# One pair of heads on GpSimd, and one probability unit, arranged anew in a fused attention and mixer kernel

## What is computed

```python
q_rot, k_rot = rotate(q), rotate(k)        # x1*cos - x2*sin, x1*sin + x2*cos
scores = scale * q_rot @ k_rot.T
attn = exp(scores - max(scores)); attn = attn / (sum(attn) + 1e-9)
x = attn @ v                               # all heads side by side: [4, 576, 512]
x = gated mixer(x; w_k, w_v, w_r)
x = token mixer and channel mixer(x; w_tok1, w_tok2, w_ch1, w_ch2)
```

## Time and profile before

| | us |
|---|---|
| median of 3 runs | 1166.11 (1163.17 to 1166.35) |
| the profiled execution | 1165.27 |
| its span in the profile | 1163.1 |
| first P0 that waits, head 2, to P0 of head 31: 29 slots | 28.42 to 476.35 |
| one slot, the mean | 15.45 |

### The profile page before, as it was taken

How to read it: one execution, slowest core, us unless ns; L and a number is a source line. 1 busy time by engine, 2 the same in 40 slices (tenths; PEclk the granted TensorE clock), 3 DMA queues, 4 the chain that set the end, 5 groups by cost and what they waited for, 6 DMA issues and landing times.

```text
span 1163.1 us, 21141 instructions
## 1 busy us (share of the span) xinstructions
PE 1016.8 (87%) x6976; PEld 961.7 (83%) x6976; DVE 636.4 (55%) x1232; ACT 537.0 (46%) x1280; POOL 298.0 (26%) x291
## 2 busy tenths in 40 slices
PE   4877777777777777879999999999999999999998
PEld 3766666666776666779999999988899999999997
DVE  5666666667666666779777777744522122212211
ACT  3666666666666666764444434435312112211210
POOL 4454555554544455442000000024200000000000
PEclk9888888998888888889999999999999999999999
DMA  3122222222222121111000000003000000000000
GB/s 81 38 60 58 60 57 52 53 60 60 60 42 42 40 39 31 22 47 62 1 0 0 0 0 0 0 28 108 28 1 21 21 1 20 20 20 0 20 20 20
DMA packets 93629, 37.70 MB, mean 32 GB/s; under 512 B 84000, under 2 KB 84896, under 8 KB 93600
## 3 DMA queue, kind: packets, MB, share of 16 engines
q1 hardware_dynamic: 93312, 37.00, 12.9%
q10 hardware_dynamic: 288, 0.33, 0.1%
HBM read 32.51 MB, written 4.80 MB: 32 GB/s over the span
## 4 chain that ended last, share of the span: by engine, by line
PE 66%; issue 14%; POOL 11%; ACT 5%; DVE 3%; POOLq 0%; DMA 0%; ACTq 0%; SPq 0%; DVEq 0%
PE psum L635 17%; PE psum L637 17%; PE psum L636 17%; PE psum L588 4%; POOL times_cos L481 3%; POOL times_sin L482 3%; PE psum L620 3%; PE psum L606 3%; POOL w_lo L501 2%; PE psum L572 2%; PE psum L626 2%; ACT probs L837 1%; ACT pT_hi L850 1%; POOL rot_q L486 1%; PE psum L723 1%
## 5 line engine op out<-in xcount | busy, mean ns | idle before, releaser
L1054 DVE TENSOR_REDUCE neg_max<-psum 128x1 f32<-128x576 f32 (+1 forms) x160 | 120.5, 753 | 120.8 <-PE psum L588 112.0
L1003 ACT ACTIVATE h_hi<-psum 128x288 fp32r<-128x288 f32 x96 | 39.5, 411 | 245.8 <-PE psum L637 245.8
L606 PE MATMUL psum<-ident,probs 128*128 128x128 f32 x800 | 137.9, 295 | 2.4 <-issue 2.3
L572 PE MATMUL psum<-ident,rot_q 128*128 128x128 f32 x96 | 24.7, 387 | 117.6 <-issue 109.1
L850 ACT ACTIVATE pT_hi<-psum 128x320 fp32r<-128x320 f32 (+3 forms) x224 | 100.7, 450 | 42.7 <-PE psum L606 38.9
L837 ACT ACTIVATE probs<-psum,neg_max 128x576 f32<-128x576 f32 (+1 forms) x160 | 118.0, 737 | 3.6 <-DVE neg_max L1054 2.0
L606 PEld LDWEIGHTS psum<-ident,probs 128*128 128x128 f32 x800 | 103.3, 151 | 17.9 <-issue 8.6
L588 PE MATMUL psum<-kT_hi,qT 128*128 128x288 f32 x320 | 111.3, 360 | 7.4 <-DVE kT_lo L1038 5.6
L572 PEld LDWEIGHTS psum<-ident,rot_q 128*128 128x128 f32 x96 | 14.4, 192 | 123.7 <-issue 123.7
L635 PE MATMUL psum<-u_hi,wc_hi 128*128 128x288 f32 x384 | 114.3, 298 | 0.2 <-DVEq L1239 0.2
L635 PE MATMUL psum<-h_hi,wc_hi 128*128 128x288 f32 x384 | 113.7, 296 | 0.0
(11 more groups left out here) (127 smaller groups left out, 2943.0 us busy)
## 6 DMA issues: line engine op xcount, KB each, us to landing
stage_w<-in_moe_w_ch_dram SPq DMA_DIRECT2D x8, 768.0 KB, 4.2
rb<-sum_rows SPq DMA_DIRECT2D x32, 144.0 KB, 3.6
out_dram<-stage_out SPq DMA_DIRECT2D x8, 576.0 KB, 3.7
raw_qk<-in_q_dram SPq DMA_DIRECT2D x32, 128.0 KB, 2.5
raw_qk<-in_k_dram SPq DMA_DIRECT2D x32, 128.0 KB, 2.3
raw_v<-in_v_dram SPq DMA_DIRECT2D x32, 128.0 KB
w_raw<-in_moe_w_k_dram SPq DMA_DIRECT2D x4, 512.0 KB, 5.0
w_raw<-in_moe_w_v_dram SPq DMA_DIRECT2D x4, 512.0 KB, 4.9
```

The lines of the kernel that those rows point to most:

```text
L572: t.transpose(prep_bank[:, p * P:(p + 1) * P], rot_q[i][:, 2 * p:2 * p + 2, :].rearrange("p a d -> p (a d)"), ident[:, :])
L606: ins = t.transpose(bank[:, at:at + P], probs[i][:, tile, at_key:at_key + P], ident[:, :])
L1054: d_.tensor_reduce(neg_max[0:m, at:at + 1], score_banks[at][0:m, :, 0:HALF], AX.XY, ALU.max, negate=True).then_inc(maxed, 1)
```

## The change

GpSimd's order in a pair becomes: rotation of head 2 it + 2, weights hi, split of the values of head 2 it, rotation of head 2 it + 3, weights lo, scaling of the pair before, split of the values of head 2 it + 1. `split_w1_hi` asks for `it` weight loads and no longer for `it + 1` (a piece is half a load). `WHOLE` is empty: unit 0 is split as the other seven are, so that each slot has an L0 (VectorE) and V0 is four FP32R matmuls. The three orders of a slot are written anew.

```diff
-    WHOLE = (0,)
+    WHOLE = ()
...
-    ORDER = steps("T0 T1 S0 P0 S1 T2 V0 T3 V1 S2 T4 V2 T5 S3 P1 T6 V3 T7 S4 V5 V4 V6 V7")
+    ORDER = steps("S0 T0 T1 S1 P0 T2 T3 V0 S2 T4 V1 T5 V2 S3 P1 T6 T7 V3 S4 V4 V6 V5 V7")
...
-    DVE_ORDER = steps("I0 M0 L0 L1 M1 P0 L2 P1 L3 M2 P2 L4 O0 L5 M3 L6 L7 M4 P3 O1")
+    DVE_ORDER = steps("M0 I0 L0 L1 M1 L2 P0 L3 M2 P1 P2 L4 L5 O0 M3 L6 L7 P3 M4 O1")
...
             def slots(it, n, scaling):
-                split_v(it, 0, 0)
                 rotate(it, 0, 2, False)
                 split_w1_hi(it, n)
+                split_v(it, 0, 0)
                 pool.wait_ge(w_hi, it + 1)
-                split_v(it, 1, 1)
+                rotate(it, 1, 3, False)
                 split_w1_lo(it)
-                rotate(it, 1, 3, False)
                 if scaling:
                     scale_x(it - 1)
+                split_v(it, 1, 1)
...
-                slots(it, it + 1, True)
+                slots(it, it, True)
...
-                if n == WHOLE[-1]:
+                if n == 0:
```

More of the change, by code:

```diff
@@ L60, in steps @@
         return [(x[0], int(x[1])) for x in text.split()]
-    ORDER = steps("T0 T1 S0 P0 S1 T2 V0 T3 V1 S2 T4 V2 T5 S3 P1 T6 V3 T7 S4 V5 V4 V6 V7")
-    ACT_ORDER = steps("H0 H1 P0 P1 P2 H2 E0 H3 E1 H4 O0 H5 E2 v0 H6 H7 P3 E3 O1 E4")
-    DVE_ORDER = steps("I0 M0 L0 L1 M1 P0 L2 P1 L3 M2 P2 L4 O0 L5 M3 L6 L7 M4 P3 O1")
+    ORDER = steps("S0 T0 T1 S1 P0 T2 T3 V0 S2 T4 V1 T5 V2 S3 P1 T6 T7 V3 S4 V4 V6 V5 V7")
+    ACT_ORDER = steps("H0 H1 E0 H2 P0 P1 H3 P2 E1 H4 v0 H5 O0 E2 H6 H7 P3 E3 O1 E4")
+    DVE_ORDER = steps("M0 I0 L0 L1 M1 L2 P0 L3 M2 P1 P2 L4 L5 O0 M3 L6 L7 P3 M4 O1")
     LAST_ORDER = steps("T0 T1 V0 V1 T2 T3 V2 T4 V3 K0 T5 V4 K1 T6 V5 K2 T7 V6 K3 V7")
```

## The result

| | us | ratio to the kernel before |
|---|---|---|
| before, median of 4 runs | 1166.23 | |
| changed, median of 4 runs | 1100.29 (1098.07 to 1101.30) | 0.9432 (0.9404 to 0.9461) |
| predicted | 1054 (1038 to 1086) | |

The direction was right and the size was not: 66 us gained where 112 were forecast, and the time lies above the forecast range. The profiled execution of the changed kernel took 1101.3 us, its span is 1099.3.

A forecast was written before the change was run, and what follows sets the result against it. GpSimd and the attention slot waited for each other, 15.45 us a slot; then VectorE would bind at 11.7. 29 x (15.45 - 11.7) = 108.8, plus 3.4, less 0.7, is 111.5 us saved: 1054, range 1038 to 1086.

The forecast's parts named there:

- a ring of waits: Attention slot: P0, v0, split of the values, rotation, next P0; 15.45 us a slot, whole wait at P0 claimed gone.
- the turn that you forecast: Attention slot without the wait at P0, as long as VectorE needs: floor 11.08 plus 0.6 idle, 11.7 us (11.1 to 12.3).

## What to carry to other kernels

When a ring of waits is cut, the next one is the longest of all the rings, those through the queue that issues transfers included: list that queue's own waits and its issues for one turn, and compare the sum with the turn that you forecast. A wait for a store's landing in an in-order queue belongs behind every load that doesn't need it (some 40 us here, and nothing in the kernel before, where another ring was longer). Look also at when the loads next to such a store come in, and not only at when they were issued. Compare variants on one chip only: here 19 us of difference between two runs of one program looked like the price of three different edits.

## What the runs showed of the hardware

- A store of 2.5 KB in elements of 4 bytes, from 128 partitions, took 8.3 to 11.9 us in the changed kernel until it could be read back, and a fifth of the elements still 7.9 on the average, where the loads of q and k, of 128 KB each, landed after 2.3 to 2.5 us (median) in the kernel before. Why so much of it is fixed stays open.
- Loads issued within about a microsecond of that store were slow with it: the values, issued right behind it, reached ScalarE 7.2 to 11.5 us after the last was issued, and q and k, issued 0.7 us ahead of it, GpSimd after 12.5 at 231.58.
- The mean differed from chip to chip: 9.3 to 9.4 us on four, 9.9 on that of the result, 11.7 in a kernel with the loads behind the store where another chip had 10.6. Four to ten runs of a kernel on a chip agree within 1%, so it isn't noise between executions; its cause stays open.
- An addition of a constant to 5 elements a partition on VectorE took 0.16 us with GpSimd idle and up to 1.60 beside its instructions, nearly always until the end of one; the reciprocal of the same elements 0.17 to 0.19 always.
